# A convolution and two expert layers on one core: the first slot on both row tiles, and where the weights are cast

## What is computed

```python
# conv: out[b,s,h,g] = sum_k softmax(weight)[h,k] * x_pad[b, s+k, h, g]
h = x @ w_in          # layer 1
g = h * np.cos(h)
x = g @ w_out
h = x @ w_in2         # layer 2
g = h * np.clip(h + 3.0, 0.0, 6.0) / 6.0
return (g @ w_out2).astype(np.float32)
```

## Time and profile before

| | |
|---|---|
| time, median of 3 runs | 2235.36 us (2234.8 to 2235.38) |
| the profiled execution | 2235.08 us, its span 2233.4 us |
| PE / PEld busy | 2224.2 (100%) / 2084.0 us (93%), 19492 each |
| DVE busy | 1825.6 us (82%) |
| ACT busy | 1734.1 us (78%) |
| POOL busy | 1510.6 us (68%) |
| L467, L474, L481 matmuls | 386 ns each of 9216, 6144 and 4096 in all |
| g_lo (L1160), g_hi (L744) | 1456 and 631 ns, x1024 |
| pre (L732), gate (L919), layer 2 | 685 and 679 ns, x512 |
| fraction (L905), cosine (L740), layer 1 | 686 and 720 ns, x512 |

### The profile page before, as it was taken

The page is one execution under the profiler, slowest core; times in us unless marked ns, Lnnn a source line. Parts: engine busy times, 40 slices in busy tenths (PEclk is TensorE's granted clock), DMA queues, the critical chain, the costliest instruction groups (busy, mean ns, idle before and its releaser), DMA issues.

```text
span 2233.4 us, 56647 instructions
## 1 busy us (share of the span) xinstructions
PE 2224.2 (100%) x19492; PEld 2084.0 (93%) x19492; DVE 1825.6 (82%) x2497; ACT 1734.1 (78%) x2846; POOL 1510.6 (68%) x1067
## 2 busy tenths in 40 slices
PE   9999999999999999999999999999999999999999
PEld 7899999999999999999999999999999999999998
DVE  8988888888888888888888888888888888888754
ACT  8788777787777877778877788777787777877775
POOL 7976666666666666766666666666666666666665
PEclk9999999999999999999999999999999999999999
DMA  4200000000000000000000000000000000000001
GB/s 107 55 8 16 15 10 4 14 14 14 14 0 14 14 14 14 0 14 14 14 14 7 7 14 14 14 13 1 14 14 14 14 0 14 14 14 7 4 6 23
DMA packets 208556, 33.14 MB, mean 15 GB/s; under 512 B 203136, under 2 KB 207232, under 8 KB 208512
## 3 DMA queue, kind: packets, MB, share of 16 engines
q1 hardware_dynamic: 205344, 32.14, 8.1%
q10 hardware_dynamic: 3168, 0.39, 0.1%
HBM read 19.92 MB, written 12.58 MB: 15 GB/s over the span
## 4 chain that ended last, share of the span: by engine, by line
PE 97%; DVE 1%; ACT 1%; issue 0%; DVEq 0%; ACTq 0%
PE h_ps L467 46%; PE acc L474 30%; PE acc_tail L481 20%; DVE gate L916 0%; PE acc_tail L699 0%; ACT pre L740 0%; ACT pre L730 0%; ACT g_hi L744 0%; PE h_ps L691 0%; DVE wtail_hi L1027 0%; DVE pre L905 0%; PE acc L598 0%; DVE in_tail L1051 0%; ACT in_tail L767 0%; DVE win_hi L1027 0%
## 5 line engine op out<-in xcount | busy, mean ns | idle before, releaser
L1160 POOL TENSOR_TENSOR g_lo<-gate,g_hi 128x512 fp32r<-128x512 f32 x1024 | 1469.6, 1456 | 702.3 <-ACT g_hi L744 701.9
L474 PE MATMUL acc<-g_hi,wout 64*128 64x512 f32 x4096 | 1416.4, 386 | 0.0
L467 PE MATMUL h_ps<-in_hi,win_hi 64*128 64x512 f32 x2048 | 790.1, 387 | 1.5 <-DVE in_tail L1051 1.3
L481 PE MATMUL acc_tail<-g_lo,wout 64*128 64x512 f32 x2048 | 790.8, 386 | 0.0
L481 PE MATMUL acc_tail<-g_hi,wout 64*128 64x512 f32 x2048 | 790.7, 386 | 0.0
L474 PE MATMUL acc<-g_lo,wout 64*128 64x512 f32 x2048 | 790.4, 386 | 0.0
L467 PE MATMUL h_ps<-in_lo,win_hi 64*128 64x512 f32 x2048 | 790.2, 386 | 0.0
L467 PE MATMUL h_ps<-in_tail,wtail_hi 64*128 64x512 f32 x2048 | 789.3, 386 | 0.6 <-DVE in_tail L1051 0.6
L467 PE MATMUL h_ps<-in_hi,win_lo 64*128 64x512 f32 x2048 | 789.4, 386 | 0.0
L474 PEld LDWEIGHTS acc<-g_hi,wout 64*128 64x128 f32 x4096 | 753.5, 184 | 27.0
L744 ACT ACTIVATE g_hi<-gate 128x512 fp32r<-128x512 f32 x1024 | 623.8, 631 | 116.2 <-DVE gate L919 56.7
(11 more groups left out here) (116 smaller groups left out, 2339.1 us busy)
## 6 DMA issues: line engine op xcount, KB each, us to landing
out_dram<-o_blk SPq DMA_DIRECT2D x128, 64.0 KB, 1.8
x_in<-in_x SPq DMA_DIRECT2D x126, 64.0 KB, 2.2
blk_tail<-in_x SPq DMA_DIRECT2D x62, 64.0 KB, 2.2
out_dram<-blk_tail SPq DMA_DIRECT2D x62, 64.0 KB, 1.8
stage<-in_moe_w_out SPq DMA_DIRECT2D x7, 384.0 KB, 3.3
stage<-in_moe_w_in SPq DMA_DIRECT2D x3, 512.0 KB, 4.0
stage<-in_moe_w_in SPq DMA_DIRECT2D x6, 256.0 KB, 4.2
pre<-in_moe_w_in SPq DMA_DIRECT2D x2, 256.0 KB, 4.5
```

The source lines that it names most:

```text
L467: return pe.matmul(chunk_of(h_ps, q, half), w, x, start=start, stop=stop)
L474: return pe.matmul(acc[pair][:, :], wout[layer][rows, 2 * q + half, cols], g[rows, :], start=start, stop=stop)
L481: return pe.matmul(acc_tail[pair][:, :], wout[layer][rows, 2 * q + half, P:2 * P], g[rows, :], start=start, stop=stop)
L1160: pool.tensor_tensor(chunk_of(g_lo, q, half), chunk_of(gate, q, half), chunk_of(g_hi, q, half).bitcast(F32), ALU.subtract).then_inc(glo_re ...
```

## The change

- Slot 0 (`slot_0`): lower and upper row tile at once, each on the other half's chunk, then traded; two last single matmuls. The waits of TensorE on itself are `lower_part` and `upper_part`.
- The main channels of tile 1 are convolved by VectorE alone; its first two taps run ahead of phase 1, behind the turn of its x and the low split of the tails. `convolve_second` and the two diagonals for it go.
- The tails' taps are spread first, and ScalarE copies them out; the turn of both tails comes ahead of the copy of the main taps. The four ones matmuls behind the spreading go.
- The second half of layer 1's input weights comes as four pieces of 512 columns in place of two of 1024, so there are 20 pieces; buffer 3 holds a main and a tail piece side by side.
- The casts: VectorE has six in phase 1 (four before) and three in phase 2 (five before), ScalarE five in phase 3 (three before), and one within slot 0 in place of ahead of it. `LOW_IN` follows.
- ScalarE keeps tile 1's halo in slot 3 (slot 0 before), VectorE makes the low tail of tile 1 in slot 4 (slot 2 before).

```diff
-WARM_BEHIND = 2
-                  Piece(0, OUT, 0, QUARTER, 2, 0, 4), Piece(0, IN, W, FF, 3, 0, 5),
-                  Piece(0, IN_TAIL, W, FF, 4, 0, 6), Piece(0, OUT, QUARTER, 2 * QUARTER, 3, 0, 5),
+                  Piece(0, OUT, 0, QUARTER, 2, 0, 4), Piece(0, IN, W, W + TOK, 3, 0, 5),
+                  Piece(0, IN_TAIL, W, W + TOK, 3, TOK, 7), Piece(0, OUT, QUARTER, 2 * QUARTER, 4, 0, 6),
+                  Piece(0, IN, W + TOK, FF, 3, 0, 5), Piece(0, IN_TAIL, W + TOK, FF, 3, TOK, 7),
                   Piece(0, OUT, 2 * QUARTER, 3 * QUARTER, 4, 0, 6), Piece(0, OUT, 3 * QUARTER, CHUNKS, 3, 0, 5),
-        LOADED_FIRST = 7
+        LOADED_FIRST = 8
-            return max(a for a in range(n) if PIECES[a].flag == PIECES[n].flag)
+            return max(a for a in range(n) if PIECES[a].buf == PIECES[n].buf and columns_of(a) & columns_of(n))
-        FIRST_PIECE_OF = {0: {0: 1, 2: 3, 4: 6}, 2: {0: 11, 4: 13}}
-        OUT_PIECES = {0: [4, 7, 8, 9], 2: [14, 15, 16, 17]}
-        HIGH_BY_DVE = {0: {0: 6, 1: 7, 3: 8, 5: 9}, 1: {0: 10, 1: 11, 2: 12, 4: 13, 7: 14}}
-        HIGH_IN = {2: {0: 15, 2: 16, 4: 17}}
+        FIRST_PIECE_OF = {0: {2: 3, 4: 6, 6: 9}, 2: {0: 13, 4: 15}}
+        OUT_PIECES = {0: [4, 7, 10, 11], 2: [16, 17, 18, 19]}
+        HIGH_BY_DVE = {0: {0: 6, 1: 7, 2: 8, 3: 9, 5: 10, 6: 11}, 1: {0: 12, 1: 13, 2: 14}}
+        HIGH_IN = {2: {0: 15, 1: 16, 3: 17, 4: 18, 6: 19}}
+        HIGH_BETWEEN = 5
-        LOW_IN = {1: 6, 2: 7, 4: 8, 6: 9, 8: 10, 10: 11, 12: 12, 14: 13, 16: 14, 18: 15, 20: 16, 22: 17}
+        LOW_IN = {1: 6, 2: 7, 3: 8, 4: 9, 5: 10, 7: 11, 8: 12, 10: 13, 12: 14, 16: 15, 17: 16, 19: 17, 20: 18, 22: 19}
-        SECOND_BY_PE, THIRD_BY_ACT = 2, {2: 0, 7: 1}
+        THIRD_BY_ACT = {2: 0, 7: 1}
+        CONV_BEFORE = 2
-        KEEP_1, TWIN_1, TAIL_1, LOW_TAIL_1, HIGH_1, LOW_1 = 0, 1, 2, 2, 5, 6
+        KEEP_1, TWIN_1, TAIL_1, LOW_TAIL_1, HIGH_1, LOW_1 = 3, 1, 2, 4, 5, 6
...
-                pe.matmul(h_ps[:, 0, 0:TAPS], head_of[:, 0:P], w_soft[:, :], start=True, stop=True)
                 pe.matmul(h_ps[:, 1, 0:TAPS], head_of[:, P:D + DT], w_soft[:, :], start=True,
+                          stop=True).then_inc(taps_spread, 1)
+                pe.matmul(h_ps[:, 0, 0:TAPS], head_of[:, 0:P], w_soft[:, :], start=True,
                           stop=True).then_inc(taps_spread, 1)
...
+            def slot_0(ph):
...
+                for n in (0, 2, 1):
+                    split_waits(n)
+                    low, up = lower_0(0, n, start=n == 0), upper_0(1, n, start=n == 0)
+                low.then_inc(lower_part, 1)
+                up.then_inc(upper_part, 1)
+                pe.wait_ge(upper_part, 1)
+                pe.wait_ge(lower_part, 1)
+                for n in (0, 2, 1):
+                    low, up = lower_0(1, n), upper_0(0, n)
+                low.then_inc(lower_part, 1)
+                up.then_inc(upper_part, 1)
+                pe.wait_ge(upper_part, 2)
+                pe.wait_ge(lower_part, 2)
+                for n in (3, 4):
+                    split_waits(n)
+                    low, up = lower_0(0, n), upper_0(1, n)
+                low.then_inc(lower_part, 1)
+                up.then_inc(upper_part, 1)
+                pe.wait_ge(lower_part, 3)
+                upper_0(0, 3, stop=True).then_inc(h_ready, 1)
+                pe.wait_ge(upper_part, 3)
+                pe.wait_ge(h_ready, 1)
+                lower_0(1, 3, stop=True).then_inc(h_ready, 1)
...
-                if 0 < q <= SECOND_BY_PE and i == 4:
-                    convolve_second(q - 1)
...
-            ones_times_ones(WARM_BEHIND)
...
                     before_gate(ph.layer, q, slot)
+                    if ph.setup == 0 and q == 0:
+                        weight_high(HIGH_BETWEEN)
...
-            act.wait_ge(taps_ready, 2)
+            act.wait_ge(taps_spread, 1)
+            act.activation(taps[:, TAIL, :], h_ps[:, 1, 0:TAPS], ACT.Copy).then_inc(tail_taps_ready, 1)
+            act.wait_ge(tail_taps_ready, 1)
...
-            for t in range(SECOND_BY_PE):
-                act.activation(diagonal_main(t), eye, ACT.Copy, scale=taps[:, MAIN, t:t + 1]).then_inc(diag_ready, 1)
...
-            for n in (4, 5):
-                weight_high(n)
+            weight_high(4)
...
-            dve.wait_ge(taps_spread, 1)
-            dve.tensor_copy(taps[:, TAIL, :], h_ps[:, 1, 0:TAPS]).then_inc(taps_ready, 1)
+            turn_two_tails()
+            dve.wait_ge(taps_spread, 2)
             dve.tensor_copy(taps[:, MAIN, :], h_ps[:, 0, 0:TAPS]).then_inc(taps_ready, 1)
-            turn_two_tails()
             turn_main(0)
-            dve.wait_ge(taps_ready, 2)
+            dve.wait_ge(taps_ready, 1)
+            dve.wait_ge(tail_taps_ready, 1)
             for t in range(TAPS - 1):
                 conv_first(0, t)
             conv_first_last()
             split_low_first()
             dve.wait_ge(halo_ready, 5)
             turn_main(1)
+            split_low_tail(acc_tail[1][0:DT, :], L2, 0)
+            for t in range(CONV_BEFORE):
+                conv_first(1, t)
             phase(first_phase())
```

More of the change, by code:

```diff
@@ L184, in conv_moe_kernel @@
         o_stored = sem("o_stored")
-        staged = [sem(f"staged{n}") for n in range(7)]
+        staged = [sem(f"staged{n}") for n in range(8)]
         whi_done = sem("whi_done")
@@ L199, in conv_moe_kernel @@
         diag_ready = sem("diag_ready")
-        second_begun = sem("second_begun")
+        tail_taps_ready = sem("tail_taps_ready")
+        lower_part = sem("lower_part")
+        upper_part = sem("upper_part")
         third_begun = sem("third_begun")
@@ L239, in staged_by, with columns_of @@
             return 16 * sum(len(loads_of(a)) for a in range(n + 1) if PIECES[a].flag == PIECES[n].flag)
+        def columns_of(n):
+            p = PIECES[n]
+            return set(range(p.at, p.at + (QUARTER * D if p.kind == OUT else p.stop - p.start)))
         def before_in_buffer(n):
-            return max(a for a in range(n) if PIECES[a].flag == PIECES[n].flag)
+            return max(a for a in range(n) if PIECES[a].buf == PIECES[n].buf and columns_of(a) & columns_of(n))
         def every_other(a, rows, odd):
@@ L362, in steps_before @@
                 return TAPS * i
-            return len(STEPS) * (i - 1) - SECOND_BY_PE - (0 if isinstance(i, int) and i == 2 else len(THIRD_BY_ACT))
+            return len(STEPS) * (i - 1) - (0 if isinstance(i, int) and i == 2 else len(THIRD_BY_ACT))
         def splits_convolved(ph, q):
@@ L484, in source_waits @@
             def source_waits(ph, q):
-                if q == 0 and ph.setup == 0:
-                    return
                 if ph.setup in FIRST_PIECE_OF and q in FIRST_PIECE_OF[ph.setup]:
@@ L525, in first_lower @@
                     pe.wait_ge(g_ready, 2 * slot - 3 + half)
-                if ph.setup == 0 and q == 0 and half == 0:
-                    split_waits(n)
                 last = first_unit(LOW, ph.layer, ph.source, q, half, n, start=n == 0)
@@ L535, in first_upper @@
                 if n == 0:
-                    pe.wait_ge(h_lower, 2 * slot + half + 1)
+                    pe.wait_ge(h_lower, 2 * slot + half - 1)
                 last = first_unit(UP, ph.layer, ph.source, q, half, n, stop=i in (3, 8))
@@ L591, in mix_of, with lower_0, upper_0 @@
                 return None if ph.setup == 0 else (ph.before, 1 - pair_of(ph), q - LAG + SLOTS)
[L593 to L601, removed]
+            def slot_0(ph):
+                def lower_0(half, n, start=False, stop=False):
+                    return first_unit(LOW, L1, ph.source, 0, half, n, start=start, stop=stop)
+                def upper_0(half, n, start=False, stop=False):
+                    return first_unit(UP, L1, ph.source, 0, half, n, start=start, stop=stop)
+                for n in (0, 2, 1):
[21 more added lines that the diff above has]
+                lower_0(1, 3, stop=True).then_inc(h_ready, 1)
             def rest_of_upper(i, ph, q):
-                if 0 < q <= LAG and i < 4:
+                if 1 < q <= LAG and i < 4:
                     first_upper(5 + i, ph, q - 1, ph.base + q - 1)
-                if 0 < q <= SECOND_BY_PE and i == 4:
-                    convolve_second(q - 1)
             def alone(ph, q):
@@ L620, in phase @@
                 for q in range(SLOTS):
+                    if ph.setup == 0 and q == 0:
+                        slot_0(ph)
+                        continue
                     if ph.setup == 0 and q < LAG:
@@ L790, in tap_third @@
             def tap_third(n):
+                act.wait_ge(taps_ready, 1)
                 act.wait_ge(halo_ready, 4 * 2 + 2)
@@ L991, in conv_first @@
             def conv_first(i, t):
[L993 to L998, removed]
+                if t > 0:
+                    dve.wait_ge(conv_step, steps_before(i) + t)
                 else:
-                    dve.wait_ge(x_turned, 1)
+                    dve.wait_ge(x_turned, i + 1)
```

3 lines of the change are left out of this document (removed).

## The result

The changed kernel takes 2240.51 us (median of 16 runs, 2238.97 to 2242.38) where the kernel before took 2235.47 beside it: ratio 1.0022, interval 1.0015 to 1.003. It is slower by 5.0 us; 2238.1 was forecast, in a range of 2232.6 to 2240.8. Its profiled execution took 2241.01 us with a span of 2239.3, 5.9 above the span of before.

A forecast was written before the change was run, and what follows sets the result against it. TensorE, with 97% of the chain, was taken to bound the kernel. +2.3 us at slot 19 (containing slot 8's +0.3 and slot 16's -1.4) and +0.7 at slot 21 gave +3.0: 2238.1 us, range 2232.6 to 2240.8.

The forecast's parts named there:

- Bound and pace: Whole kernel: TensorE holds 97% of the chain at 0.2266 us a turn; nothing changes behind the third of 64 phases.
- The tails' start and slot 0: Start: first tail tap 0.65 us earlier at about 5.6, slot 0 at 13.4, first pre at 16.5, 0.85 earlier.
- The casts of phase 1: Slots 5 to 8: VectorE's six casts delay low 10 and in_lo, using up the start's gain; slot 8 +0.3 us.
- Phase 2: Slots 12 to 16: without the tail cast in_tail is no longer late; slot 16 at 82.3, gain 1.4 us.
- Phase 3: Slots 16 to 21: low 16 comes late behind GpSimd's six operations (8.2 us); slot 19's mix 2.3 later, slot 21 another 0.7.
- Rival 1: Phase 3: the low parts are in time and slot 16's 1.4 us gain stays, 2233.7 us; chance 0.27.
- Rival 3: Phase 3: VectorE's taps slow GpSimd's six operations to 1.65 us each, 2240.4 us; chance 0.12.
- rival 4: Start: the clock rises only after the tails, costing 4.3 us, 2242 us; chance 0.06.
- The wait in slot 21: Slot 21: mix waits for the low part of piece 17, cast at the end of slot 19; 0.7 us (0.2 to 1.3).
- The sum: Up to slot 24: +2.3 at slot 19 and +0.7 at slot 21, +3.0 us; own range 2235.7 to 2240.3.

The follow-up runs named there:

- the kernel with the start alone: Kernel before with only the new slot 0, tile 1's taps on VectorE and the tails first; old pieces, casts and low parts: 2235.69 us, ratio 1.0.
- With slot 7 and in_lo mended: Changed kernel with piece 15 cast by VectorE, low parts reordered, piece 10 cast in slot 4, slot 6's in_lo ahead of the cast: 2235.75 us, 1.0001.
- second execution: Profiled execution of the unmodified changed kernel, measured again as a yardstick: median 2240.1 us, ratio 1.002.
- the two experiments with the low parts put back: Changed kernel with pieces 15 and 16 cast by VectorE in phase 2, 2236.59 us; or only piece 15, with low 16 ahead of g_lo 16, 2236.8 us.
- the one with the tail's piece back: Changed kernel with piece 15 cast by VectorE in slot 12, pieces 16 to 19 on ScalarE, low 16 ahead of g_lo 16: 2236.8 us, 1.0005.
- the filler kernel: Changed kernel with 12 matmuls on one row tile ahead of slot 19's wait for low 16: 2239.2 us, on another chip 2239.53 us.

## Why the prediction was right, and where its size was off

**Bound and pace: right.** TensorE's pace didn't move, and all of the difference lies ahead of slot 24.

**The tails' start and slot 0: right.** 5.54 against 5.6, and 13.39 against 13.4, in the execution that was profiled, where the clock rose at 8.9 as before. The first pre came at 16.91, not 16.5: the single upper matmul before it started at 16.31, not 16.05, since the groups of pairs followed each other 0.50 to 0.54 apart where I had 0.46 and each group's first pair took 0.1 more than a turn; and pre followed 0.60 behind it, not 0.45.

**The casts of phase 1: right in the total, with a wait left out.** The low part that slot 7 needs was done at 44.54 (44.0 forecast), TensorE waited 0.60 and slot 8 was at 48.15 (47.9). The cast ahead of in_lo took 1.38, within the two ends of the earlier trace rows, and in_lo started behind it at 47.38. But the larger wait of this stretch, 1.45 in slot 6 for the low part of the new, smaller tail piece 9, isn't in my sum. It didn't show in the total since slot 8 was held by in_lo and the gates anyway. From slot 0 to slot 8 it is 34.8 us here, and 34.1 in the kernel with the start alone (no smaller pieces, no such wait). With slot 7 and in_lo mended it is 34.1 too, and the wait of slot 6 is still there. That speaks against a price of its own; the wait alone was not taken away.

**Phase 2: the mechanism right, its size subject to chance.** Slot 16 was forecast at 82.3; the profiled execution had 84.00, the second one 82.87. Neither waits for in_tail, as forecast; the first waits 0.89 for in_twin, which ScalarE made at 83.11, behind the late gates. (The 82.3 was worked out for a slot 8 that is level; with the +0.3 forecast there it would be 82.6. The total doesn't change by it.) The first difference between the two executions is one tiny copy of six columns. In the profiled one:

```profile
60.08 1.34 DVE L1008 COPY halo<-xT 128x6 f32<-128x6 f32 x1
61.33 1.34 DVE L1007 COPY xT_tail<-halo_tail 64x6 f32<-64x6 f32 x1
```

Beside GpSimd's group of g_lo these take 1.34 each, where the copy just before them took 0.16; in the other execution only the second was held (1.27), as in the execution of before. The gate behind them was at 64.79 in the one and at 63.48 in the other, and slot 16 is 1.1 apart. The Trainium skill (SBUF — State Buffer, "Who interferes with whom") says that a VectorE copy of this sort and a GpSimd operation exclude each other for a whole instruction. By that rule the size of the copy doesn't matter, and the trace agrees: six columns took as long as the cast of 768 at 46.08.

**Phase 3: right, and the main term nearly so.** Forecast: slot 16 to the mix of slot 19 in 17.4 us, of which 3.66 lost; measured 17.1, lost 3.35. GpSimd's six operations took 8.4 (8.2 taken). The second execution has the same 17.1 and 8.4. The cast on ScalarE ended at 92.55, not 91.2, which is less than the 1.7 by which slot 16 was late. Rival 1 fell, and the two experiments with the low parts put back say why: GpSimd's g_lo took about as long (1.61 us in the one with the tail's piece back, 1.65 here), but there was less in its queue ahead of low 16. Rival 3, GpSimd at 1.65 for each operation, did not occur either: 8.4 / 6 = 1.40.

**The term that was missing: the clock.** My rival 4 looked for the clock at the start, where it cost nothing in the profiled execution. It came back in slot 19, behind the very wait that I forecast. TensorE stood 3.4 us from start to start, the clock was at its half level from 101.1 to 104.5, and 16 turns took 5.1 us. I had the length of the wait and did not ask what the engine is worth after it: the sum has this term at nothing, and it measured 1.5. The Trainium skill (TensorE: Matmul & The Clock Gate, "What's actually happening") says that idling brings the half level back, and that the moment at which the clock rises varies from run to run. The runs here agree with both: the fall stands behind 3.0 us of idling, and with the same start the rise lay between 8.8 and 10.4 us. The wait in slot 21 was 0.43 idle, 0.6 against the pace (0.7 forecast).

**The sum**, step by step, forecast and measured in the profiled execution: to slot 8 +0.3, +0.55; slot 8 to 16 -1.7, -0.2; to the mix of 19 +3.7, +3.4; clock 0, +1.5; slot 21 +0.7, +0.6. Together +3.0, +5.8. Without the clock's fall that is 4.3, 2239.4 us, and the filler kernel, which had no fall in a trace, measured 2239.2 and 2239.5; with it 2240.9. In the second execution the mix of slot 19 stands 2.6 over before, where 2.3 was forecast, so that without the clock the sum would be +3.2. The 16 runs, sorted by their mean granted clock, lie on both: the five with 1.000 have a median of 2239.6, the nine with 0.999 have 2241.0, the two with 0.998 took 2240.3 and 2242.4. That mean also takes in the clock's rise at the start, so it is no count of the falls: of the 27 runs of before beside the changed kernel's second turn, those with 0.999 were the shorter ones (2235.1 against 2236.1), and the trace of before has no fall. The order is a hint and no proof.

**How much was luck.** The measured 2240.5 lies inside the stated range, 0.3 under its upper end, and just outside the 2235.7 to 2240.3 that the sum gave for itself. It also lies on rival 3's 2240.4, though GpSimd at 1.65, rival 3's mechanism, did not occur. The stated range reached that far because of rival 3, and not because anything in it allowed for a fall behind the wait.

**Still open.** What decides in one execution whether the clock falls behind the 3.0 us wait, and whether one copy of slot 10 or two collide, isn't settled. That the filler prevents the fall rests on three traces without a fall against two of three with one, and on a difference of 0.9 us; both, fall and collision, differ between executions of the same or nearly the same code.

## To carry to other kernels

A cast on one in-order engine and its subtraction on another are one chain: before moving the first, count what the second engine has queued between it and the consumer. A gain at the start ends at the first fixed due time behind it (here in_lo in slot 6), so move that too, or count the gain as nothing. Where a change leaves TensorE idle for some us, price the half clock behind the wait as well; if the wait has to stay, matmuls into a bank that is about to be overwritten kept the clock up in three traces of three.

## What the runs showed of the hardware

- Behind an idle stretch of TensorE of 3.0 us (3.4 from start to start) the granted clock fell to its half level for 3.4 us in two of three profiled executions (the changed kernel twice, and the one with two ones matmuls more, where it didn't); the matmuls started 0.43 apart in place of 0.227. With 12 matmuls in the stretch it didn't fall in any of three, and the median beside the changed kernel was 0.9 us lower.
- At the start the clock rose between 8.8 and 10.4 us in eleven executions of kernels that start alike on TensorE, and slot 0 came with it at 13.3 to 14.1, so that it alone can move slot 0 by 0.8 us. In the one execution with two ones matmuls more it rose at 11.0, slot 0 at 14.6.
- Copies of six columns on VectorE took 0.15 or 0.16 us where they were not held, and 1.27 to 1.34 where they were, each one by itself, while GpSimd ran its g_lo.
- Passing a bank from one row tile to the other took TensorE 0.50 to 0.54 us from start to start, with turns at 0.227.
